# First values of the second layer's semaphores, the bank of its tile 1, and the place of the tile-count read

## What is computed

```python
scores = (1 / S) * z @ z.T                     # 4 batches, S = 2496, 64 wide
x = u * (maximum(scores, 0) ** 2 @ v)
# layer one: rows with x @ w_skip > 0 take part, the others pass through
e = argmax(x @ w_gate); g = softmax(x @ w_gate)[e]
x = x + g * (maximum(x @ w1[e], 0) @ w2[e])    # 8 experts, F = 1024
# layer two: every row
logits = x @ w_gate2 + modality_bias[modality_id]
e = argmax(logits); g = softmax(logits)[e]
out = g * (maximum(x @ w1b[e], 0) @ w2b[e])
```

## Time and profile before

| what | value |
|---|---|
| runs | 1476.66, 1475.3, 1475.42 us; median 1475.42 |
| the profiled execution | 1478.75 us |
| its span, first to last instruction | 1477.2 us |
| PE busy | 1454.6 us, 98% of the span |
| DVE, ACT, POOL busy | 66%, 53%, 19% |
| granted TensorE clock | 0.998 |
| layer one's loop begins, layer two begins | 725.0 us, 1002.8 us |

### The profile page before, as it was taken

How to read it: one execution, slowest core, us unless ns; L and a number is a source line. 1 busy time by engine, 2 the same in 40 slices (tenths; PEclk the granted TensorE clock), 3 DMA queues, 4 the chain that set the end, 5 groups by cost and what they waited for, 6 DMA issues and landing times.

```text
span 1477.2 us, 34369 instructions
## 1 busy us (share of the span) xinstructions
PE 1454.6 (98%) x11832; PEld 1312.6 (89%) x11832; DVE 980.9 (66%) x2487; ACT 778.2 (53%) x1540; POOL 278.9 (19%) x309
## 2 busy tenths in 40 slices
PE   9999999999999999999999999999999999999997
PEld 7889998999998898889899999997888888888885
DVE  7988888888788888888676666674333333333332
ACT  6677767677667677666444444444333333333332
POOL 4011111111111111111332222225121121211212
PEclk9999999999999999999999999999999999999999
DMA  5311030201311111031464344323111121111110
GB/s 122 101 52 45 30 101 29 66 31 43 101 63 39 38 50 67 31 102 58 131 211 131 129 142 133 107 97 124 47 43 47 40 73 43 43 47 40 58 44 26
DMA packets 59066, 108.01 MB, mean 73 GB/s; under 512 B 18615, under 2 KB 33474, under 8 KB 58940
## 3 DMA queue, kind: packets, MB, share of 16 engines
q1 hardware_dynamic: 40396, 47.46, 11.5%
q0 software_dynamic: 18544, 58.96, 11.4%
HBM read 75.61 MB, written 32.31 MB: 73 GB/s over the span
## 4 chain that ended last, share of the span: by engine, by line
PE 95%; issue 2%; DVE 1%; ACT 0%; DMA 0%; SPq 0%; POOLq 0%; DVEq 0%; POOL 0%; ACTq 0%
PE pO L1578 33%; PE pS L1886 11%; PE pO L1894 10%; PE pS L1567 9%; PE pS L1851 9%; PE pO L1834 9%; PE pO L1896 5%; PE pM L1886 4%; PE pT L1877 1%; PE pO L1587 1%; PE pM L1650 1%; DVE AH L1183 1%; PE pT L1769 1%; PE pO L1751 0%; PE pS L1738 0%
## 5 line engine op out<-in xcount | busy, mean ns | idle before, releaser
L1578 PE MATMUL pO<-AH,VH 64*128 64x512 f32 (+1 forms) x1520 | 323.8, 383 | 0.8 <-DVE AL L1185 0.5
L1578 PE MATMUL pO<-AH,VL 64*128 64x512 f32 (+1 forms) x1520 | 322.9, 382 | 1.7 <-issue 1.7
L1578 PE MATMUL pO<-AL,VH 64*128 64x512 f32 (+1 forms) x1520 | 323.1, 382 | 0.0
L742 ACT ACTIVATE R<-pS 128x512 f32<-128x512 f32 (+1 forms) x400 | 213.7, 589 | 168.3 <-PE pS L1567 165.6
L1185 DVE TENSOR_TENSOR AL<-A,AH 128x512 fp32r<-128x512 f32 (+1 forms) x400 | 278.9, 697 | 13.7
L751 ACT ACTIVATE A<-R 128x512 f32<-128x512 f32 (+1 forms) x400 | 228.2, 626 | 9.0 <-DVE AL L1185 9.0
L1894 PE MATMUL pO<-VL,AH 128*128 128x512 f32 x640 | 232.2, 400 | 0.0
L1183 DVE CAST AH<-A 128x512 fp32r<-128x512 f32 (+1 forms) x400 | 170.5, 426 | 45.7 <-ACT A L751 45.2
L1578 PEld LDWEIGHTS pO<-AH,VH 64*128 64x128 f32 x1520 | 172.2, 184 | 15.8 <-issue 1.5
L1578 PEld LDWEIGHTS pO<-AH,VL 64*128 64x128 f32 x1520 | 172.4, 184 | 15.2 <-issue 2.9
L1578 PEld LDWEIGHTS pO<-AL,VH 64*128 64x128 f32 x1520 | 172.4, 184 | 12.5
(11 more groups left out here) (276 smaller groups left out, 2387.4 us busy)
## 6 DMA issues: line engine op xcount, KB each, us to landing
raw<-in_w_dram POOLq DMA_DIRECT2D x22, 1024.0 KB
A<-token_rows SPq DMA_DIRECT2D x20, 536.0 KB
uT<-in_u_dram SPq DMA_DIRECT2D x16, 512.0 KB, 3.7
xin<-token_rows SPq DMA_DIRECT2D x23, 268.0 KB
raw<-in_v_dram SPq DMA_DIRECT2D x8, 768.0 KB
A<-in_w2t_dram POOLq DMA_DIRECT2D x8, 512.0 KB
raw<-in_z_dram SPq DMA_DIRECT2D x8, 368.0 KB, 5.0
token_rows<-pad_row SPq DMA_DIRECT2D x8, 268.0 KB
```

Source lines behind the costliest of these rows:

```text
L742: s_.activation(R[k % 2][:, 0:n], pS[k % 2][:, 0:n], ACT.Relu, scale=1.0 / S).then_inc(relu_done, 1)
L1578: last = t_.matmul(pO[:, (KD * r + d) * QW:(KD * r + d) * QW + n], vv[rows, vo + k * D + d * P:vo + k * D + (d + 1) * P], a[k % NBUF][rows ...
```

## The change

1. DVE gives `PH[1].h_split` its first 8 and `PH[1].y_out` its first 1 at the lead section of layer one, together with those of `PH[0]`, and no longer at the start of `second_phase`.
2. Tile 1 of layer two is turned in the bank pM instead of pT, by PE, ACT and DVE alike. PE therefore waits for `PH[0].base` (`place_tile` has read the prefix counts) instead of `q.h_split` at NF + 7.
3. `lead_layer2(3, 3)` stands ahead of PE's wait for `cum_ready` and the read `first_end`.

```diff
--- before.py
+++ after.py
@@ -942,8 +942,8 @@
                     h_high(0, f, hring_lead)
                     if 3 <= f < 3 + WP:
                         split_high(E + 1, 1, f - 3)
-                take_half(1, 0, 0, pT[:, :])
-                take_half(1, 0, 1, pT[:, :])
+                take_half(1, 0, 0, pM[:, :])
+                take_half(1, 0, 1, pM[:, :])
                 keep_marks(1, 0)
                 act.wait_ge(marks_loaded, 16)
                 for s in range(SUB2):
@@ -1302,7 +1302,9 @@
                 ins.then_inc(gpart_low, 1)
 
             dve.sem_inc(PH[0].h_split, 4)
-            dve.sem_inc(PH[0].y_out, 1)
+            dve.sem_inc(PH[1].h_split, NF)
+            for q in PH:
+                dve.sem_inc(q.y_out, 1)
             dve.wait_ge(u_loaded, 16 * CHUNKS)
             for d in range(KD):
                 sum_rows(CHUNKS, d).then_inc(o_summed, 1)
@@ -1462,8 +1464,6 @@
             def second_phase():
 
                 q = PH[1]
-                dve.sem_inc(q.h_split, NF)
-                dve.sem_inc(q.y_out, 1)
 
                 def low_half(t, par, kd, bank):
 
@@ -1500,8 +1500,8 @@
                 finish_groups(1)
                 for f in range(3, NF):
                     h_low(0, f, hring_lead)
-                low_half(1, 0, 0, pT[:, :])
-                low_half(1, 0, 1, pT[:, :])
+                low_half(1, 0, 0, pM[:, :])
+                low_half(1, 0, 1, pM[:, :])
                 dve.wait_ge(marks_loaded, 16)
                 add_parts(0, 1)
                 total = dve.value_load(cum[0:1, 1, E:E + 1], min_val=0, max_val=64)
@@ -1795,9 +1795,9 @@
                 lead_layer2(1, 2)
                 gate_columns(1)
                 lead_layer2(2, 1)
+                lead_layer2(3, 3)
                 pe.wait_ge(cum_ready, ph + 1)
                 first_end = end_of(pe, 0, 0)
-                lead_layer2(3, 3)
 
                 def prefix_x2(idx):
                     pe.wait_ge(q.onehot, idx)
@@ -1932,9 +1932,10 @@
                     layer1(0, 1, 0, f, hring_lead)
                 layer1(0, 1, 0, NF - 1, hring_lead)
                 layer2(0, 0, 4)
-                pe.wait_ge(q.h_split, NF + 7)
-                transpose_half(1, 0, pT)
-                layer2_last(0, 0, lambda: transpose_half(1, 1, pT))
+                pe.wait_ge(PH[0].base, total0 + 1)
+                pe.sem_inc(pe_passed, 1)
+                transpose_half(1, 0, pM)
+                layer2_last(0, 0, lambda: transpose_half(1, 1, pM))
                 pe.wait_ge(cum_ready, 2)
                 total = pe.value_load(cum[0:1, 1, E:E + 1], min_val=0, max_val=64)
```

## The result

The change makes the kernel slower. On the chip of the runs before, it takes 1478.73 us (median of 14 runs, 1476.92 to 1479.44) against 1475.34 us (14 runs, 1474.45 to 1476.66): a ratio of 1.0022, 95% interval 1.0015 to 1.0029. I had forecast 1475.1 us with a range up to 1476.3. The profiled execution of the changed kernel took 1478.61 us.

What follows compares the result with a forecast made beforehand. The prediction took PE as the bound, with 95% of the chain. Gains of 0.2 (part 1), 0 (part 2) and 0.1 us (part 3) made 0.3, so 1475.42 became 1475.1 us, range 1473.4 to 1476.3.

Steps and rivals of the forecast that it cites:

- the wait of 1.34 us: PE's idle time before layer two's first matmul, released by DVE's semaphore values; part 1 aimed to remove it.
- I had said 0.2: Part 1's forecast gain at the prefix counts: 0.2 us, the rest returning as a wait for the one-hot table.
- The step that failed: Tile 1's load hangs on the same DVE chain as the one-hot table, so it was to come 0.2 us sooner.
- gaps: Pauses of PE among layer one's lead-tile matmuls near the tile-count read, 1.6 us beyond regular spacing; doubted in timed runs.
- its largest price for "slower" was 0.6 us: Ahead of layer one's loop, the late read could leave PE without queued matmuls, costing up to 0.6 us.
- three signs of being wrong: Prefix counts not waiting; transposes within 0.2 us of the preceding matmul; runs over 2 us faster despite the one-hot wait.
- the value of 0.1 us: Part 3's forecast gain at the start of layer one's loop, assuming no pauses among the lead-tile matmuls.
- The 1.1 us: Time from the branch into layer one's loop to its first matmul, 723.9 to 724.99, counted as sequencer work.
- the 1.3 us that the forecast quotes: A skill page's TENSOR_LOAD time for PE's count read; it would make loop entry another 1.0 us later.
- my first rival: Layer one's lead-tile pauses come from the count read and occur in timed runs: 1473.7 us, chance 15%.
- the third rival: Slower: the late read leaves PE bare ahead of layer one's loop, up to 0.6 us, giving 1475.8; chance 10%.
- 3.3 us of profiling: Whole kernel: profiled execution 1478.75 us against median run 1475.42, so some 3.3 us were taken as absent from other runs.

Runs made afterwards that it cites:

- e1: Only the second layer's semaphore first values moved earlier, against the kernel before: 1472.97 us against 1470.54, ratio 1.0015.
- e4: The changed kernel plus GpSimd waiting for layer two's tile counts before making low parts of weights: 1470.39 us, 0.9998 of the kernel before.
- e5: The changed kernel itself, measured again on another chip against the kernel before: 1472.66 us against 1470.42, ratio 1.0012.
- e6: The changed kernel plus 32 short PE matmuls of constants while PE waits for tile 1: 1471.42 us, 1.0004 of the kernel before.
- e11: Kernel before plus part 1, with both halves of tile 1 turned later, without an added GpSimd wait: 1469.41 us against 1470.59, ratio 0.9992.
- e2: Only tile 1's bank changed, pM for pT, with its wait, against the kernel before: 1470.66 us, ratio 1.0001.
- e3: Only the read of the tile counts moved behind lead_layer2(3, 3), against the kernel before: 1470.50 us, ratio 1.0000.
- e9: Kernel before plus part 1, GpSimd's wait for the tile counts, tile 1 turned later and weights asked for later: 1468.87 us against 1470.59, ratio 0.9988.
- e7: The kernel before with two extra SyncE reads of a tile count ahead of tile 1's load: 1472.32 us, 1.0014 of the kernel before.
- e10: The kernel before with one extra SyncE read of a tile count ahead of tile 1's load: 1471.37 us against 1470.59, ratio 1.0009.
- e8: Kernel before plus part 1, GpSimd's wait for the tile counts, and tile 1's halves turned later: 1469.73 us against 1470.42, ratio 0.9994.

## Why the prediction was wrong

**Part 1.** Right up to the prefix counts: block f = 1 waited for the copy (0.3 us), the counts for the one-hot table (0.6 us), and the counts came only 0.36 us sooner (4.54 to 4.18 in the table). From start to start the wait of 1.34 us was worth 1.49, and 1.1 of it came back. I had said 0.2. DVE's chain did move by 0.19 us (10.63 to 10.44); the rest is that PE, when it already waits, starts 0.06 us after the one-hot table is written and not 0.24.

**The step that failed** is the sentence "so that the load too comes 0.2 us sooner. That is part 1's gain, passed on rather than lost". I followed DVE's chain and took the durations of its instructions as given. But ScalarE's high parts of the weights follow PE, and GpSimd's low parts follow ScalarE. Part 1 moved PE by 0.36 us, GpSimd's start by 0.36 (10.78 to 10.42) and DVE by 0.19, and the 0.15 us between the write of the counts and GpSimd's start was gone: GpSimd now starts just ahead of it (1009.33 against 1009.35). The write took 1.29 us and not 0.17, and the load was issued 0.8 us later, not 0.2 us sooner. e1 shows that the timing of part 1 is enough for it, e4 that GpSimd is the cause. The row of GpSimd right behind the write stood in the trace of before; I did not look at which engines ran beside the chain. The Trainium skill states the rule for it, page "SBUF — State Buffer", section "Who interferes with whom": VectorE and GpSimd share one pair of ports, some VectorE operations lock it, and whoever comes second is blocked until the other's instruction ends. The rows of after, e1, e5, e6 and e11 agree (1.23 to 1.30 us beside one GpSimd instruction of 1.28 or 1.29, 0.17 when it starts after). That ports are what is shared no run here shows.

**The clock** was nowhere in my sum. I priced a later load by its lateness. e6 separates the two: about 1 us for lateness, and 1.2 us between the medians for the clock; where it fell in the profile, 3.4 us at half clock cost 1.6. The forecast had no rival with either mechanism, and its largest price for "slower" was 0.6 us. None of its three signs of being wrong came true either; what did not fit was in its other statements, that the transposes would wait about 1.2 us (2.2) and come 0.2 us closer to layer one's end (0.6 us further).

**Part 2.** Right: the transposes waited for the load, not for the bank, and e2 finds nothing (1.0001).

**Part 3.** Where there are no gaps the value of 0.1 us was right within what can be measured (e3, 1.0000), but by luck. The forecast has the sequencer set the start of the loop in both orders, with 1.1 us from the branch to the first matmul. In e2 and e3 PE set it: the branch is issued 14.3 us behind the lead tile's first matmul in e2 and 15.2 in e3, not 0.1 us sooner but 0.9 later, and the loop starts at 16.51 in both, since matmuls were still queued. The 1.1 us were read where PE was not idle either; where it was, in after, 0.78 us passed (721.84 to 722.62). PE's read of the counts took 0.5 us in e1 to e11 and 0.57 and 0.68 in the first two profiles, so the 1.3 us that the forecast quotes did not occur.

The gaps were not the read's: they stayed in the changed kernel ahead of the moved read, which settles my first rival against it. Timeline of PE, after, as the earlier trace rows (the first two gaps, 0.23 and 0.32 us, are at 719.29 and 720.02; the read begins at 720.80):

```profile
720.75 0.37 PE L1738 MATMUL pS<-VL,AL 128*128 128x264 f32 x1 [0.45 <-issue]
...
722.62 0.50 PE L1834 MATMUL pO<-ZH,VH 128*128 x2 [0.78 <-issue]
```

The idle time ahead of the loop was 0.78 us and not 0.3. In before the gaps stood behind the read and gave the sequencer time; now they stand ahead of it. In these two profiles the loop starts 0.48 us later with the change than without (19.01 against 18.53 us behind the lead tile's first matmul). That is the third rival, the late read that leaves PE bare, close to its price of 0.6 us. Whether it is in the timed runs of that chip too no run shows.

**The timed runs and the profile.** I took the profiled execution as 3.3 us of profiling. The changed kernel's profiled and timed executions agree (1478.61 and 1478.73), and no profile of e1 to e11 has the gaps from 690 us on. So they are not a constant price of profiling. What makes them is open. Open too is why the change costs 3.4 us in the result and 2.2 in e5. That the clock falls more often there (13 of 14 runs in the upper group against 7 of 11) does not explain it, since both medians lie in the upper group. The 0.48 us of part 3 may be a part of it; and the intervals of the two ratios overlap.

## What to carry to other kernels

A chain on one engine that moves by tenths of a microsecond also moves against every engine beside it: before costing a move, list what GpSimd does during the VectorE instructions that something waits for, and how much time lies between them. Price a wait of PE by its idle time and by the clock behind it, and check whether it can be filled with work that is there anyway, as in e9; that gained 1.7 us where the three parts of this change, each alone, gained nothing measurable or lost. And when a transfer is needed sooner, see what else is on the DMA engines then.

## What the runs showed of the hardware

- A VectorE write of 128 x 9 values took 1.23 to 1.30 us when a GpSimd subtraction of 128 x 512 had started 0.02 to 0.08 us earlier (after, e1, e5, e6, e11), and 0.17 us when it started 0.14 us or more later. Beside the same subtraction a VectorE instruction of 128 x 512 with one of its inputs in PSUM took its usual 0.69 us (before, 1011.96).
- TensorE's granted clock fell to 1.2 GHz for 3.4 us behind an idle time of 2.2 us (after) and 2.7 us (e1), 0.3 and 1.3 us after PE had started again; it stayed at 2.4 GHz behind 2.2 us (e5), 2.9 us (e7) and 1.9 us (e10). By the groups of times it fell in 8 of 11 runs of e1, 7 of e5, and 4 each of e7 and e10. With 32 short matmuls in that wait (e6) the 11 runs are one group.
- A load of 536 KB took 3.7 us alone (before, tile 1) and 8.5 us beside a 2 MB load of weights (e8, tile 2).
- Three gaps in a row among PE's matmuls, of 0.2 to 0.45 us idle each, occurred behind the short matmuls of layer one's lead tile in both profiles from one chip, and in none of the eleven from three others.
